# Second-layer weights split into high and low parts during the first layer, kept in DRAM, and loaded at the change of layers

## What is computed

```
scores = scale * q_c @ concat(mem_k, k[l_start:r_end]).T
out_c  = softmax(scores) @ concat(mem_v, v[l_start:r_end])
```

```
h = x @ w_in            # 512 x 2048
x = max(0.01*h, h) @ w_out      # first layer
h = x @ w_in2
P = a0 + a1*h + a2*h^2 + a3*h^3
Q = 1 + |b0|*|h| + |b1|*h^2
out = (P / (Q + 1e-6)) @ w_out2   # second layer
```

## Time and profile before

| | |
|---|---|
| median of 3 runs | 1173.3 us (1172.52 to 1176.18) |
| the profiled execution | 1174.36 us |
| its span in the profile | 1172.6 us |
| granted TensorE clock | 0.999 |
| busy: TensorE, weight load, VectorE, ScalarE, GpSimd | 98%, 92%, 62%, 48%, 11% of the span |
| moved by DMA | 81.19 MB, mean 69 GB/s |

### The profile page before, as it was taken

One profiled execution on the slowest core, in us unless ns is written; L12 is line 12 of the kernel. 1 busy time (PEld: TensorE's weight loads), 2 busy tenths in 40 slices (PEclk: granted clock), 3 DMA queues, 4 the chain that ended last, 5 costly groups with the idle time before them and its releaser, 6 DMA issues.

```text
span 1172.6 us, 23562 instructions
## 1 busy us (share of the span) xinstructions
PE 1153.5 (98%) x9077; PEld 1080.6 (92%) x9077; DVE 724.7 (62%) x1363; ACT 563.0 (48%) x1154; POOL 130.0 (11%) x132
## 2 busy tenths in 40 slices
PE   8999999999999999999998999999999999999998
PEld 7999999999999999999997899999999899999996
DVE  4554434434334344433338888888887888888886
ACT  2323223232222232322225667676766767676765
POOL 5960000000000000000399000000000000000000
PEclk9999999999999999999999999999999999999999
DMA  7652212213122032200445102020200102020000
GB/s 284 206 162 80 66 46 101 73 40 109 61 100 69 23 127 64 82 19 2 175 131 154 44 1 82 1 81 1 82 1 31 52 0 81 0 81 1 28 1 28
DMA packets 24583, 81.19 MB, mean 69 GB/s; under 512 B 2848, under 2 KB 2976, under 8 KB 24480
## 3 DMA queue, kind: packets, MB, share of 16 engines
q1 hardware_dynamic: 24480, 79.77, 20.1%
HBM read 60.89 MB, written 18.87 MB: 68 GB/s over the span
## 4 chain that ended last, share of the span: by engine, by line
PE 94%; DVE 2%; issue 1%; DMA 1%; ACT 0%; POOL 0%; SPq 0%; DVEq 0%; ACTq 0%
PE psum L412 15%; PE psum L414 15%; PE psum L413 15%; PE psum L427 8%; PE psum L429 7%; PE psum L428 7%; PE psum L446 7%; PE psum L447 7%; PE psum L445 7%; PE psum L382 1%; PE psum L360 1%; PE psum L392 1%; PE psum L368 1%; PE psum L399 1%; DMA raw<-weights_in 1%
## 5 line engine op out<-in xcount | busy, mean ns | idle before, releaser
L412 PE MATMUL psum<-x_hi,w_hi 128*128 128x384 f32 x1024 | 343.7, 336 | 1.4 <-issue 1.4
L414 PE MATMUL psum<-x_hi,w_lo 128*128 128x384 f32 x1024 | 344.0, 336 | 0.0
L413 PE MATMUL psum<-x_lo,w_hi 128*128 128x384 f32 x1024 | 343.0, 335 | 0.0
L719 DVE TENSOR_TENSOR scratch<-psum,scratch 128x384 f32<-128x384 f32 x128 | 71.4, 558 | 273.2 <-ACT scratch L565 272.5
L565 ACT ACTIVATE scratch<-psum 128x384 f32<-128x384 f32 x128 | 63.0, 492 | 291.3 <-PE psum L414 290.3
L412 PEld LDWEIGHTS psum<-x_hi,w_hi 128*128 128x128 f32 x1024 | 192.3, 188 | 8.0 <-issue 2.2
L413 PEld LDWEIGHTS psum<-x_lo,w_hi 128*128 128x128 f32 x1024 | 192.2, 188 | 5.4
L414 PEld LDWEIGHTS psum<-x_hi,w_lo 128*128 128x128 f32 x1024 | 192.2, 188 | 0.0
L427 PE MATMUL psum<-g_hi,w_hi 128*128 128x384 f32 x512 | 179.4, 350 | 0.1
L428 PE MATMUL psum<-g_lo,w_hi 128*128 128x384 f32 x512 | 171.7, 335 | 0.0
L429 PE MATMUL psum<-g_hi,w_lo 128*128 128x384 f32 x512 | 171.6, 335 | 0.0
(11 more groups left out here) (59 smaller groups left out, 1442.5 us busy)
## 6 DMA issues: line engine op xcount, KB each, us to landing
scratch<-groups_in SPq DMA_DIRECT2D x24, 768.0 KB, 5.1
raw<-weights_in SPq DMA_DIRECT2D x64, 256.0 KB, 2.7
scratch<-groups_in SPq DMA_DIRECT2D x24, 512.0 KB, 4.0
x_hi_scratch<-x_hi SPq DMA_DIRECT2D x8, 768.0 KB, 3.7
x_lo_scratch<-x_lo SPq DMA_DIRECT2D x8, 768.0 KB, 5.6
x_hi<-x_hi_scratch SPq DMA_DIRECT2D x8, 768.0 KB, 4.4
x_lo<-x_lo_scratch SPq DMA_DIRECT2D x8, 768.0 KB, 5.9
out<-scratch SPq DMA_DIRECT2D x24, 256.0 KB, 2.2
```

Source lines behind the costliest of these rows:

```text
L412: nc.tensor.matmul(bank, hi, x_hi[:, b, k, :], start=(k == 0), stop=False)
L413: nc.tensor.matmul(bank, hi, x_lo[:, b, k, :], start=False, stop=False)
L414: last = nc.tensor.matmul(bank, lo, x_hi[:, b, k, :], start=False, stop=(k == KT - 1))
```

## The change

Two DRAM scratches hold the second layer's weights already split. `raw` halves 32 to 63 are loaded in tiles 1 to 5 of phase A (two per attention group, behind its loads), split by GpSimd into `w2_high` (two buffers) and, in place, `raw`; SP stores both. At the change GpSimd does nothing: SP loads the high and the low part of each half straight into w_hi and w_lo, and TensorE waits for these loads. To make room for `w2_high`, `first` now lies over the place of w_hi from slice 14 on, so GpSimd waits for the first tile's attention before half 28. The core of the diff (waits in gemm1, gemm2_a and gemm2_b go through wait_weights; the arguments `w_base` go):

```diff
+    w2_hi = nc.dram_tensor("w2_hi_scratch", [HALVES, P, D_MODEL], F32, kind="Internal").ap()
+    w2_lo = nc.dram_tensor("w2_lo_scratch", [HALVES, P, D_MODEL], F32, kind="Internal").ap()
...
+    FIRST_F = 14
+    with contextlib.ExitStack() as early:
+        early.enter_context(nc.sbuf_tensor("before_first", [P, FIRST_F, 2, D_MODEL], F32))
+        first = early.enter_context(nc.sbuf_tensor("first", [P, 3 * 512], F32))
...
-    first = sb("first", [P, 3 * 512], F32)
+    w2_high = sb("w2_high", [P, 2, D_MODEL], F32)
...
+            def load_raw2(k, r):
+                sp.wait_ge(w2_stored[r], 8 * (k - r) + 1)
+                sp.dma_start(raw[:, r, :], weights[bass.ds(k + HALVES, 1), :, :].rearrange("a p n -> (a p) n")
+                             ).then_inc(raw_loaded[r], 16)
+            def store_w2(k, r):
+                sp.wait_ge(w2_split, k + 1)
+                sp.dma_start(w2_hi[bass.ds(k, 1), :, :].rearrange("a p n -> (a p) n"), w2_high[:, r % 2, :]
+                             ).then_inc(w2_stored[r], 16)
+                sp.dma_start(w2_lo[bass.ds(k, 1), :, :].rearrange("a p n -> (a p) n"), raw[:, r, :]
+                             ).then_inc(w2_stored[r], 16)
+            def keep_w2(k, r):
+                store_w2(k, r)
+                load_raw2(k + 2, (r + 2) % RAW)
+            def load_w2(j):
+                sp.wait_ge(h_ready if j % 2 == 0 else g_used, STEPS_A - NF + j // 2 + 1)
+                for dst, src in ((w_hi, w2_hi), (w_lo, w2_lo)):
+                    sp.dma_start(dst[:, j // 2, j % 2, :].bitcast(F32), src[j, :, :]).then_inc(w2_loaded[j], 16)
...
             load_group(7, 7)
+            for r in range(RAW):
+                sp.sem_inc(w2_stored[r], 1)
+            sp.wait_ge(w_ready, HALVES)
+            load_raw2(0, 0)
+            load_raw2(1, 1)
             with sp.Fori(0, 2) as i:
                 for c in (0, 1):
                     store_y(2 * i + c, c)
                     for e in range(GPT):
                         load_group(6 * i + 8 + 3 * c + e, 8 + 3 * c + e)
+                        for u in (0, 1):
+                            at = 6 * c + 2 * e + u
+                            keep_w2(12 * i + at, at % RAW)
             store_y(4, 0)
             for g in (20, 21, 22):
                 load_group(g, g)
+                for k in (2 * g - 16, 2 * g - 15):
+                    keep_w2(k, k % RAW)
             store_y(5, 1)
             load_group(23, 23)
+            store_w2(30, 2)
+            store_w2(31, 3)
             store_y(6, 0)
+            for r in range(RAW):
+                sp.wait_ge(w2_stored[r], 32 * HALVES // RAW + 1)
 
             sp.wait_ge(y_stored, 32 * 7 + 1)
             load_x2(0, 0)
-            with sp.Fori(HALVES // RAW, 2 * HALVES // RAW) as i:
-                for r in range(RAW):
-                    load_raw(i * RAW + r, r)
+            for j in range(HALVES):
+                load_w2(j)
...
+                if j == 2 * FIRST_F:
+                    pool.wait_ge(x_ready, GPT)
...
+            def split_w2(k):
+                r = k % RAW
+                pool.wait_ge(raw_loaded[r], 16 * ((HALVES + k) // RAW + 1))
+                if k >= 2:
+                    pool.wait_ge(w2_stored[(k - 2) % RAW], 32 * ((k - 2) // RAW) + 32 + 1)
+                high = w2_high[:, k % 2, :]
+                nc.gpsimd.tensor_scalar(high.bitcast(F32R), raw[:, r, :], 1.0, 0.0, ALU.mult, ALU.add
+                                        ).then_inc(w2_high_ready, 1)
+                pool.wait_ge(w2_high_ready, k + 1)
+                nc.gpsimd.tensor_tensor(raw[:, r, :].bitcast(F32R), raw[:, r, :], high, ALU.subtract
+                                        ).then_inc(w2_split, 1)
...
-            for j in range(HALVES, 2 * HALVES):
-                pool.wait_ge(h_ready if j % 2 == 0 else g_used, STEPS_A - NF + j % HALVES // 2 + 1)
-                split_half(j)
+            for k in range(HALVES):
+                split_w2(k)
...
+            def wait_weights(j, second):
+                if second:
+                    pe.wait_ge(w2_loaded[j], 32)
+                else:
+                    pe.wait_ge(w_ready, j + 1)
...
-                pe.wait_ge(w_ready, w_base + 2 * f + 2)
+                wait_weights(2 * f + 1, True)
```

More of the change, by code:

```diff
@@ L21 @@
+import contextlib
 import numpy as np
@@ L132, in build @@
     w_ready = S("w_ready")
+    w2_high_ready = S("w2_high_ready")
+    w2_split = S("w2_split")
+    w2_stored = [S(f"w2_stored{r}") for r in range(RAW)]
+    w2_loaded = [S(f"w2_loaded{j}") for j in range(HALVES)]
     scores_ready = S("scores_ready")
@@ L327, in split_half @@
             def split_half(j):
-                f, half, r = j % HALVES // 2, j % 2, j % RAW
+                f, half, r = j // 2, j % 2, j % RAW
                 pool.wait_ge(raw_loaded[r], 16 * (j // RAW + 1))
+                if j == 2 * FIRST_F:
+                    pool.wait_ge(x_ready, GPT)
                 nc.gpsimd.tensor_scalar(w_hi[:, f, half, :], raw[:, r, :], 1.0, 0.0, ALU.mult, ALU.add
@@ L399, in keep_warm, with gemm1 @@
                     nc.tensor.matmul(psum[:, 7, 0:TILE], g_hi[:, 0, 0:P], g_hi[:, 0, :], start=True, stop=True)
-            def gemm1(n, f, b, w_base, wait_for_next=None):
-                pe.wait_ge(w_ready, w_base + 2 * f + 1)
+            def wait_weights(j, second):
[3 more added lines that the diff above has]
+                    pe.wait_ge(w_ready, j + 1)
+            def gemm1(n, f, b, second, wait_for_next=None):
+                wait_weights(2 * f, second)
                 if not isinstance(n, int) or n >= 2:
@@ L415, in gemm1, with gemm2_a @@
                 last.then_inc(h_ready, 1)
-            def gemm2_a(n, f, w_base, t):
-                pe.wait_ge(w_ready, w_base + 2 * f + 2)
+            def gemm2_a(n, f, t):
+                wait_weights(2 * f + 1, False)
                 pe.wait_ge(g_lo_ready, n + 1)
@@ L433, in gemm2_a, with gemm2_b @@
                 last.then_inc(g_used, 1)
-            def gemm2_b(n, f, tp, w_base, after_phase_a=False):
-                pe.wait_ge(w_ready, w_base + 2 * f + 2)
+            def gemm2_b(n, f, tp, after_phase_a=False):
+                wait_weights(2 * f + 1, True)
                 pe.wait_ge(g_lo_ready, n + 1)
@@ L467, in wait_for_next @@
                             wait_values(g0 + VALUES_AT[f], c0 + VALUES_AT[f])
-                    gemm1(n0 + f, f % NF, (tp + f // NF) % 2, HALVES if last_tile and f >= NF else 0,
+                    gemm1(n0 + f, f % NF, (tp + f // NF) % 2, last_tile and f >= NF,
                           wait_for_next)
@@ L479, in tile_a @@
                             turn_heads(g0 + TURN_AT[f], loop_att[TURN_AT[f]])
-                    gemm2_a(n0 + f - LAG, f - LAG, 0, t)
+                    gemm2_a(n0 + f - LAG, f - LAG, t)
             def tile_b(i, tp, last_tile, first_tile=False):
@@ L488, in tile_b @@
                             pe.wait_ge(x2_loaded[1 - tp], 32 * i + 32 * (tp + 1))
-                        gemm1(n0 + f, f % NF, (tp + f // NF) % 2, HALVES)
+                        gemm1(n0 + f, f % NF, (tp + f // NF) % 2, True)
                     if f == LAG and isinstance(t, int) and t == 1:
@@ L495, in tile_b @@
                         pe.wait_ge(o_saved, GPT * t - GPT)
-                    gemm2_b(n0 + f - LAG, f - LAG, tp, HALVES, after_phase_a=first_tile and f == LAG)
+                    gemm2_b(n0 + f - LAG, f - LAG, tp, after_phase_a=first_tile and f == LAG)
             pe.wait_ge(zeros_ready, 1)
@@ L529, in _ @@
             for f in range(LAG):
-                gemm1(f, f, 0, 0)
+                gemm1(f, f, 0, False)
             with pe.Fori(0, TILES // 2 - 1) as i:
```

## The result

| | before | changed |
|---|---|---|
| median, first comparison | 1173.11 us | 1165.25 us (1165.09 to 1168.01, 5 runs) |
| ratio and 95% interval | | 0.9931 [0.9917, 0.9945] |
| a second comparison, later | 1174.94 us | 1166.28 us (5 runs), 0.9931 [0.9917, 0.9945] |
| profiled execution, its span | 1174.36, 1172.6 us | 1165.09, 1163.3 us |

The change makes the kernel 0.69% faster, 7.9 us by the first medians.

A forecast was written before the change was run, and what follows sets the result against it. It took TensorE, busy 98%, as the bound, idling 6.4 us at the change behind VectorE delayed by GpSimd's splits. Median 1173.3 - 6.2, with nothing for the moved splits and transfers, gave 1167.1 us, range 1165.8 to 1170.6.

The forecast's parts named there:

- Part one: At the change of layers: without GpSimd's splits, TensorE's four waits on VectorE go, a gain of 6.2 us, bounds 5 and 6.4.
- The four rebuilt times: VectorE's undisturbed order at the change, rebuilt with 3.61 us steps; each beats TensorE's need by 1.6, 0.6, 0.7 and 1.5 us.
- The reserve of 0.2 us for a remainder: At the change: 0.2 us of TensorE's waits kept as remaining, since ScalarE could take some of the middle margins.
- The forecast's own range: Whole kernel: 1166.4 to 1168.6 us, from a gain of 5 to 6.4 and half a us run to run; chance 0.72.
- Part two: Splits moved into tiles 1 to 5, beside attention's tight chain: nothing lost.
- the margin reckoned at 1 us: Tile 1: the second half is split by 130.1 us, the critical L722 starts at 131.11, 1 us later.
- the ten open chains: Attention's scores-to-transposes chains GpSimd's splits might meet, two in each of tiles 1 to 5, two of them with an edge.
- Rival A: Locks return in attention: GpSimd meets L722 in many chains, 1 to 4.9 us lost, most likely near 3: 1170.1; chance 0.14.
- the bound of 4.9: Attention in tiles 1 to 5: loss if all collide, 0.98 us delays less the room: 8 x 0.41 + 2 x 0.83 us.
- Part three: SP and transfers: 128 more transfers of about 0.35 us each, and 250 GB/s of loads at the change, cost nothing.
- Rival C: Tiles 7 and 8: loads of w_hi and w_lo become the bound, 19 us lost at 120 GB/s, 1186; chance 0.04.
- Rival B: The change is bound by the step itself or transfers; half or all of 6.4 us stays, 1170 to 1173.3; chance 0.10.

The follow-up runs named there:

- experiment 1: Kernel before, GpSimd only counting the second layer's 32 raw halves and splitting none (first layer's weights stay): 1166.31 us, ratio 0.9936.
- 2: Changed kernel plus 32 idle pairs of GpSimd operations reading SBUF at the change, results unused: 1174.49 us, ratio 1.0008 against the kernel before.
- 3: Changed kernel plus 128 GpSimd memsets of 128 x 512 through the change, which read no SBUF: 1165.16 us, ratio 0.9929 against the kernel before.
- 5: Changed kernel with only the last 12 of 32 halves kept in DRAM, GpSimd splitting the first 20 at the change: 1166.56 us, ratio 0.9939.
- 4: Kernel before with the changed kernel's buffer places alone (w2_high, two scratches, first over w_hi, wait for x_ready): 1174.40 us, ratio 1.0003.
- 6: Kernel before with eight late raw loads moved ahead, so splits start some 10 us sooner, no scratch: 1169.17 us, ratio 0.9958.
- experiment 9: Changed kernel with three more idle 1.28 us tensor_tensors on GpSimd in each split from half 2 on, tiles 1 to 5: 1169.69 us, ratio 0.9965.
- 7: Changed kernel with two more unused 256 KB loads behind each pair at the change, 33.5 MB instead of 16.8: 1167.28 us, ratio 0.9937.
- experiment 10: Changed kernel once more, unaltered, against the kernel before on another occasion: 1166.28 us, ratio 0.9931.
- experiment 8: Changed kernel with five more idle 0.62 us tensor_scalars on GpSimd in each split from half 2 on, tiles 1 to 5: 1166.91 us, ratio 0.9939.

## Why the prediction was right in its mechanism and short in its size

- **Part one, the mechanism: right.** The stops were VectorE's lateness under GpSimd's reads. Taking the splits away is enough (experiment 1), putting reads back undoes it (2), writes do not (3), and only the splits that meet the long steps count (5). The places of the buffers give nothing (4). The four rebuilt times held to 0.3 us.
- **Part one, the size: this is the step that failed.** It took the idle column for the whole price, "a gain of 6.2 us, bounds 5 and 6.4", and the range rested on "below it nothing has a mechanism, as the whole idle time of the change is 6.4 us". A stop costs some 0.25 us more than the column says, shown by the stretch in the kernel before (7.39 against 6.38) and in experiments 2 (8.36 against 7.14), 4 (6.88 against 5.86) and 6 (3.04 against 2.37, with the stop that the column does not show). The working had the hint in it: TensorE took 1.63 us from the first stop's end to the second for six matmuls that start 0.23 us apart, 1.38 us in all. The reserve of 0.2 us for a remainder was not needed either. Term by term: 7.4 instead of 6.2, which alone gives 1173.3 - 7.4 = 1165.9. That is still just inside the range, whose lower end of 1165.8 has no working of its own. The forecast's own range, a gain of 6.4 and half a us from run to run, began at 1166.4; with 7.4 it begins at 1165.4. The first comparison fell another 0.65 us below the corrected sum, 0.2 us of it since the kernel before had 1173.11 and not 1173.3; the second, at 1166.28 us, did not.
- **Part two: nothing to speak of was lost, in part by luck.** In tile 1 the second half was split by 130.08 us (130.1 forecast), but load_v was issued at 119.62, 0.97 us sooner than in the kernel before. So the reload and split took 10.46 us from there and not 9.5, and L722's operation began at 130.14: the margin reckoned at 1 us was 0.06. In other chains the reload often came later, and in four of the ten open chains L722's operation was longer (0.81 to 1.40 us), where the prediction had none. What saved the forecast was the room behind it: one group alone lost 0.16 us. Rival A's price was sized well: experiment 9 lost some 3 to 4 us when the chains were really hit (most likely 3 us in the prediction), and the bound of 4.9 was not reached.
- **Part three: right.** TensorE never waited on w2_loaded, and twice the traffic changed nothing (7). Rival C is excluded here. Rival B is excluded by experiments 1 and 5, in which nothing of the 6.4 us stays.
- **What stays open.** The two comparisons give 0.69% with an interval from 0.55 to 0.83%, which is 6.5 to 9.7 us; the medians are 7.9 and 8.7 us apart. The 7.4 us shown at the change lie inside. Whether up to 1 us more belongs to the change, at the end of the kernel (experiment 10), can't be told from runs that scatter by over 1 us, and the cause of what the first comparison has beyond 7.4 us stays open with it.

## What to carry to other kernels

If a GpSimd operation reads SBUF while VectorE runs operations with two SBUF operands, look at whether VectorE is then the one that TensorE waits for; here that overlap carried nearly all of the cost. Before storing everything ahead of time, try less: moving the last 12 of the 32 splits gave the whole gain, and starting the splits 10 us sooner, with no scratch, over half of it. When a gain is sized from TensorE's stops, take the distance between two landmarks with and without them, or add some 0.25 us a stop for matmuls of this size; the idle column starts behind the end of an overlapping matmul and is too small. A range whose lower end rests on the sum of the idle column is too tight for that reason.

## What the runs showed of the hardware that I had not expected

A VectorE operation that starts second waits for what is left of GpSimd's and no longer. The changed kernel shows one case, VectorE's and GpSimd's timelines:

```profile
358.12 1.40 DVE L790 TENSOR_TENSOR g_lo<-scratch,g_hi 128x384 fp32r<-128x384 f32 x1 [0.58 <-ACT g_hi L639]
...
357.82 1.28 POOL L399 TENSOR_TENSOR raw<-raw,w_high 128x512 fp32r<-128x512 f32 x1
```

The tensor_tensor of GpSimd began 0.30 us before and lasted 1.28, so 0.98 us were left; L790 took 0.84 us longer than its 0.56. In experiment 9's worst case above GpSimd's operation of 1.30 us began at 380.33, 1.25 us were left, and VectorE's took 1.10 longer. With short GpSimd operations VectorE is seldom the loser: in experiment 8, with GpSimd busy for 161 of the 380 us from 105 to 485, only 9 of 80 operations of L722's kind in tiles 1 to 5 were longer than 0.6 us. And the DMA engines held 385 to 387 GB/s from DRAM for 46 us beside full TensorE work (experiment 7).
